# A Fourier transform ahead of two expert layers: four parity classes of the sequence index, eleven chunks instead of ten, and another order of folds

## The reference

```
X = np.fft.fft(x, axis=1)        # along the sequence, 2496 points
X = np.fft.fft(X, axis=2)        # along the features, 256 points
attn = X.real                    # (4, 2496, 256), then as 9984 rows of 256
# layer 1: logits = rows @ w_gate; every row gets one of 8 experts, at most 1248 each,
#          in the order of the largest logits; out = relu(row @ w1[e]) @ w2[e]
# layer 2: each row to its largest logit's expert, scaled by a softmax and a sigmoid gate
```

## Time and profile before

| | before |
|---|---|
| median of the runs | 1381.67 us |
| the profiled execution | 1381.85 us, of which 1380.0 us are its span |
| transform along the sequence, first to last product | 14.6 to 113.4 us |
| TensorE busy in the whole span | 93% |
| mean granted clock of TensorE | 0.929 of full speed |
| moved by the queue of SyncE in the first 60 us | 16.79 MB |

### The profile page before, as it was taken

One profiled execution on the slowest core, in us unless ns is written; L12 is line 12 of the kernel. 1 busy time (PEld: TensorE's weight loads), 2 busy tenths in 40 slices (PEclk: granted clock), 3 DMA queues, 4 the chain that ended last, 5 costly groups with the idle time before them and its releaser, 6 DMA issues.

```text
span 1380.0 us, 30713 instructions
## 1 busy us (share of the span) xinstructions
PE 1279.5 (93%) x10394; PEld 1179.9 (85%) x10395; DVE 745.8 (54%) x1994; ACT 327.8 (24%) x796; POOL 560.3 (41%) x548
## 2 busy tenths in 40 slices
PE   5999899928999998899999995999999999999996
PEld 4757788817888888789898995999999999999996
DVE  2733788896776678876445434443443433333332
ACT  0102110022322232333333321222222222222221
POOL 2800002205465656565656461421443242444411
PEclk9999755558999999999999997999999999999998
DMA  9605541003212131212222222221223122232110
GB/s 346 230 11 170 190 151 66 33 2 98 92 52 87 39 99 43 95 41 101 78 80 65 81 67 65 74 76 42 68 75 99 42 76 74 76 105 73 42 42 20
DMA packets 70729, 116.20 MB, mean 84 GB/s; under 512 B 7784, under 2 KB 50545, under 8 KB 70640
## 3 DMA queue, kind: packets, MB, share of 16 engines
q1 hardware_dynamic: 46864, 72.39, 15.7%
q0 software_dynamic: 11808, 31.03, 6.9%
q10 hardware_dynamic: 11968, 11.63, 3.0%
HBM read 81.87 MB, written 34.45 MB: 84 GB/s over the span
## 4 chain that ended last, share of the span: by engine, by line
PE 73%; DVE 11%; issue 2%; DMA 1%; ACT 1%; POOL 0%; ACTq 0%; DVEq 0%; POOLq 0%; SPq 0%
PE bank L1089 22%; PE bank L1091 21%; PE bank L1090 21%; PE bank L977 3%; PE bank L960 3%; DVE hot_r L1728 2%; PE bank L1228 1%; PE bank L1101 1%; DVE hot_q L1729 1%; DVE hot_q L1727 1%; DVE hT_low L1898 1%; DVE arena L1607 1%; DVE xT_low L1891 0%; DVE arena L1672 0%; DMA arena<-in_w2a_t 0%
## 5 line engine op out<-in xcount | busy, mean ns | idle before, releaser
L1089 PE MATMUL bank<-weights_high,hT_high 128*128 (+1 forms) x1328 | 388.4, 292 | 0.0
L1091 PE MATMUL bank<-weights_high,hT_low 128*128 (+1 forms) x1328 | 378.4, 285 | 0.0
L1090 PE MATMUL bank<-weights_low,hT_high 128*128 (+1 forms) x1328 | 377.4, 284 | 0.0
L1089 PE MATMUL bank<-xT_high,weights_high 128*128 128x256 f32 (+2 forms) x1072 | 336.4, 314 | 9.1 <-DVE xT_low L1891 4.0
L1091 PE MATMUL bank<-xT_high,weights_low 128*128 128x256 f32 (+2 forms) x1072 | 331.7, 309 | 0.0
L1090 PE MATMUL bank<-xT_low,weights_high 128*128 128x256 f32 (+2 forms) x1072 | 331.0, 309 | 0.0
L1090 PEld LDWEIGHTS bank<-weights_low,hT_high 128*128 128x128 f32 x1328 | 250.5, 189 | 0.0
L1091 PEld LDWEIGHTS bank<-weights_high,hT_low 128*128 128x128 f32 x1328 | 250.4, 189 | 0.0
L1089 PEld LDWEIGHTS bank<-weights_high,hT_high 128*128 128x128 f32 x1328 | 250.1, 188 | 0.1
L1089 PEld LDWEIGHTS bank<-xT_high,weights_high 128*128 128x128 f32 x1072 | 205.1, 191 | 24.6 <-DVE hT_low L1898 7.9
L1091 PEld LDWEIGHTS bank<-xT_high,weights_low 128*128 128x128 f32 x1072 | 204.4, 191 | 11.5
(11 more groups left out here) (256 smaller groups left out, 1438.3 us busy)
## 6 DMA issues: line engine op xcount, KB each, us to landing
arena<-middle ACTq DMA_DIRECT2D x44, 258.0 KB
spectrum<-arena SPq DMA_DIRECT2D x39, 256.0 KB, 2.2
arena<-in_w2a_t SPq DMA_DIRECT2D x8, 1024.0 KB, 5.0
raw<-in_w1a SPq DMA_DIRECT2D x8, 1024.0 KB
raw<-in_w2a SPq DMA_DIRECT2D x8, 1024.0 KB
raw<-in_w1b SPq DMA_DIRECT2D x8, 1024.0 KB
raw<-in_w2b SPq DMA_DIRECT2D x8, 1024.0 KB
arena<-in_x SPq DMA_DIRECT2D x4, 768.0 KB, 4.6
```

Of the source, the lines that this page charges most:

```text
L1089: pe.matmul(out_, a[0], b[0], start=start, stop=False)
L1090: pe.matmul(out_, a[0], b[1], start=False, stop=False)
L1091: return pe.matmul(out_, a[1], b[0], start=False, stop=stop)
```

## The change

The sequence positions are sorted by n mod 4. The even positions are split once more: positions 4j (class r = 0) and 4j + 2 (class r = 1), 3 chunks of 128 each (`EC`), and the odd positions 2j + 1 are 5 chunks (`OC`); 11 chunks in all where there were 10. A load with h = 0 holds the 6 chunks of even positions, one with h = 1 the 5 chunks of odd ones. The host lays `x`, `x_rev` and the tables out in that order, so that a partition's part of a load is one contiguous piece. (Frequencies up to an eighth of the sequence are 0 to 312, `KQ` = 313 of them; `KREST` = 312.)

A unit with h = 0 is now 3 + 3 products, 313 wide, which hold the two even classes up to frequency 312; their sum (`plus`) and difference (`minus`) are the even positions' part at k and at 624 - k. A unit with h = 1 is 5 products of the odd positions for k up to 312 and 5 for k from 313 to 624. So a pair (b, q) takes 16 products. ScalarE copies one bank for a unit with h = 0 and none for one with h = 1. VectorE does two operations behind a unit with h = 0 and four behind one with h = 1 (and the one-column one for q = 0). TensorE waits for `even` or `odd` of the load that a unit reads, no longer for both loads of a sequence. GpSimd waits for `even` of load 0 only at its load 0, where it waited for load 1's at load 0 and load 3's at load 2. The first cosine piece is loaded behind the first x load; `const` and the gate weights move from behind the fourth load to behind the sixth; `tables` moves from behind unit 7 to behind unit 12.

```
+KQ = QUARTER + 1                   # 313
+KREST = QH + 1 - KQ                # 312
+EC = QUARTER // P + 1              # 3
+OC = -(-QH // P)                   # 5
+PARTS = ((0, 2 * EC), (2 * EC, 2 * EC + OC))
+PIECE_AT = (0, 2 * EC * KQ, (2 * EC + OC) * KQ, (2 * EC + OC) * KQ + OC * KREST)
+    evens = [4 * (c * P + m) + r for r in (0, 2) for c in range(EC)]
+    return np.concatenate(evens + [2 * (c * P + m) + 1 for c in range(OC)], 1)
-        FOLDS_AT = {1: (2, 3), 3: (4,), 5: (5,), 7: (6,), 9: (7,)}
+        FOLDS_AT = {1: (2,), 2: (3,), 4: (4,), 5: (5,), 7: (6,), 8: (7,)}
+        TABLES_AT = 12
...
         @block.sync
-                sp.dma_start(xlow[:, u, 0:c1 - c0],
-                             x[b, rows].rearrange("(c p q) d -> p c q d", p=P, q=2)).then_inc(s_low[u], 16)
+                sp.dma_start(xlow[:, u, 0:c1 - c0], x[b, :, c0:c1]).then_inc(s_low[u], 16)
+                sp.dma_start(xmir[:, u, 0:c1 - c0], x_rev[b, :, c0:c1]).then_inc(s_mir[u], 16)
+                if n == 0:
+                    sp.dma_start(cosb[0], table_piece(cos_n, 0)).then_inc(s_cos[0], 16)
                 if n == 1:
-                    for h, (k0, k1) in enumerate(SPANS):
-                        for q in range(2):
-                            sp.dma_start(cosb[:, q, :, k0:k1], cos_n[:, q, :, k0:k1]).then_inc(s_cos[h], 16)
...
+                    for i in (1, 2):
+                        sp.dma_start(cosb[i], table_piece(cos_n, i)).then_inc(s_cos[i], 16)
+                    a = spot["sin"][0]
+                    sp.dma_start(sinb[0], table_piece(sin_n, 0)).then_inc(s_sin[0], 16)
+                    sp.dma_start(arena[:, a + PIECE_AT[1]:a + PIECE_AT[3]],
+                                 sin_n[:, PIECE_AT[1]:PIECE_AT[3]]).then_inc(s_sin[1], 16)
-                if n == 3:
+                if n == 5:
                     sp.dma_start(cst[:], const).then_inc(s_const, 16)
...
         @block.gpsimd
-                if n in (0, 2):
-                    pool.wait_ge(s_even, n + 2)
+                if n == 0:
+                    pool.wait_ge(s_even, 1)
...
         @block.tensor
-                if q == 0 and h == 0:
-                    pe.wait_ge(s_even, 2 * (b + 1))
-                    pe.wait_ge(s_edge, 2 * (b + 1))
-                if q == 1 and h == 0:
-                    pe.wait_ge(s_odd, 2 * (b + 1))
+                if q == 0:
+                    pe.wait_ge(s_even, 2 * b + h + 1)
+                    pe.wait_ge(s_edge, 2 * b + h + 1)
+                if q == 1:
+                    pe.wait_ge(s_odd, 2 * b + h + 1)
...
                 for r in range(2):
-                    for c in range(NC):
+                    piece, chunks_ = ((0, range(r * EC, (r + 1) * EC)), (1 + r, range(2 * EC, NC)))[h]
+                    if b == 0 and q == 0 and not (h == 0 and r):
+                        pe.wait_ge(s_cos[piece], 16)
+                    if b == 0 and q == 1 and r == 0:
+                        pe.wait_ge(s_sin[h], 16)
+                    w = KREST if piece == 2 else KQ
+                    for c in chunks_:
...
         @block.scalar
-                if n >= 3:
-                    act.wait_ge(s_seq, n - 2)
-                act.copy(half[0:m, n % 3, 0:w], bank[2 * (n % 3)][0:m, 0:w]).then_inc(s_half, 1)
+                if h == 0:
+                    if n >= 4:
+                        act.wait_ge(s_seq, n - 3)
+                    act.copy(quarter[0:m, n // 2 % 2], bank[2 * (n % 3)][0:m, 0:KQ]).then_inc(s_half, 1)
...
         @block.vector
             def joined(n):
+                if h == 0:
+                    dve.wait_ge(s_half, n // 2 + 1)
+                    dve.wait_ge(s_other_ps, n + 1)
+                    dve.tensor_tensor(add, part, two[:, 0:KQ], ALU.add)
...
+                    ins.then_inc(s_seq, 1)
+                    return
...
+                dve.wait_ge(s_half_ps, n + 1)
+                dve.tensor_tensor(to[:, 0:KQ], add, one[:, 0:KQ], ALU.add)
+                mirrored(to[:, HALF - KQ + 1:HALF - low + 1], add[:, KQ - 1:stop:-1], one[:, KQ - 1:stop:-1])
...
+                dve.wait_ge(s_other_ps, n + 1)
+                dve.tensor_tensor(to[:, KQ:QH + 1], sub[:, KREST - 1::-1], two[:, 0:KREST], ALU.add)
+                mirrored(to[:, QH + 1:QH + KREST], sub[:, 1:KREST], two[:, KREST - 2::-1]).then_inc(s_seq, 1)
-                if n == 7:
+                if n == TABLES_AT:
                     tables()
```

More of the change, by code:

```diff
@@ L204, in build_program @@
         middle = nc.dram_tensor("middle", (E * REG + W2, ROW), F32, kind="Internal").ap()
[L207 to L210, removed]
+        CP = max(b - a for a, b in PARTS)
+        sizes = [("cos", PIECE_AT[3]), ("sin", PIECE_AT[3]), ("even", NC * B * P), ("odd", NC * B * P),
+                 ("quarter", 2 * KQ), ("pad", PAD), ("seqA", B * HALF), ("seqB", B * HALF), ("xlow", 2 * CP * D), ("xmir", 2 * CP * D),
+                 ("sum", CP * D), ("dif", CP * D), ("mid_col", NC * B),
+                 ("plus", 2 * KQ), ("minus", 2 * KQ)]
         at, spot = 0, {}
@@ L222, in fft, with trig @@
             return v.rearrange(pattern, **kw) if pattern else v
[L224 to L228, removed]
-        seqA, seqB = fft("seqA"), fft("seqB")
[L230 to L234, removed]
+        def trig(name):
+            t = fft(name)
+            return [t[:, PIECE_AT[i]:PIECE_AT[i + 1]].rearrange("p (c k) -> p c k", k=KREST if i == 2 else KQ) for i in range(3)]
+        cosb, sinb = trig("cos"), trig("sin")
+        even = fft("even", "p (b c d) -> p b c d", b=B, c=NC)
+        odd = fft("odd", "p (b c d) -> p b c d", b=B, c=NC)
+        mid_col = fft("mid_col", "p (c b) -> p c b", c=NC)
+        seqA, seqB = fft("seqA"), fft("seqB")
+        xlow = fft("xlow", "p (u c d) -> p u c d", u=2, c=CP)
+        xmir = fft("xmir", "p (u c d) -> p u c d", u=2, c=CP)
+        fsum, fdif = fft("sum", "p (c d) -> p c d", c=CP), fft("dif", "p (c d) -> p c d", c=CP)
+        quarter, plus, minus = (fft(n, "p (u k) -> p u k", u=2) for n in ("quarter", "plus", "minus"))
         NST = 6
@@ L386, in build_program @@
         s_mir = [sem(f"s_mir{u}") for u in range(2)]
[L387 removed]
+        s_cos, s_sin = ([sem(f"s_{n}{h}") for h in range(w)] for n, w in (("cos", 3), ("sin", 2)))
         s_even, s_edge, s_odd = sem("s_even"), sem("s_edge"), sem("s_odd")
@@ L1499, in joined @@
                 b, q, h = work_list[n]
-                k0, k1 = SPANS[h]
-                w, m = k1 - k0, (B if q == 2 else P)
-                one, two = half[0:m, n % 3], bank[2 * (n % 3) + 1][0:m]
+                m, u = (B if q == 2 else P), n // 2 % 2
+                add, sub = plus[0:m, u], minus[0:m, u]
+                one, two = bank[2 * (n % 3)][0:m], bank[2 * (n % 3) + 1][0:m]
+                if h == 0:
+                    dve.wait_ge(s_half, n // 2 + 1)
+                    dve.wait_ge(s_other_ps, n + 1)
+                    part = quarter[0:m, u]
+                    dve.tensor_tensor(add, part, two[:, 0:KQ], ALU.add)
+                    if q == 1:
+                        ins = dve.scalar_tensor_tensor(out=sub, in0=part, scalar=-1.0, in1=two[:, 0:KQ],
+                                                       op0=ALU.mult, op1=ALU.add)
+                    else:
+                        ins = dve.tensor_tensor(sub, part, two[:, 0:KQ], ALU.subtract)
+                    ins.then_inc(s_seq, 1)
+                    return
@@ L1520, in joined @@
-                if q == 0 and h == 0:
-                    ins = dve.tensor_tensor(lastA[:, b:b + 1], one[:, 0:1], two[:, 0:1], ALU.subtract)
-                ins.then_inc(s_seq, 1)
+                dve.wait_ge(s_seq, n)
+                dve.wait_ge(s_half_ps, n + 1)
+                dve.tensor_tensor(to[:, 0:KQ], add, one[:, 0:KQ], ALU.add)
+                stop = low - 1 if low else None
+                mirrored(to[:, HALF - KQ + 1:HALF - low + 1], add[:, KQ - 1:stop:-1], one[:, KQ - 1:stop:-1])
```

84 lines of the change are left out of this document (35 added, 49 removed).

## The result

| | before | after |
|---|---|---|
| median of four runs | 1381.15 us | 1366.46 us |
| ratio, 95% interval | | 0.9892 (0.988 to 0.9905) |
| profiled execution, its span | 1381.85, 1380.0 us | 1367.67, 1365.9 us |
| first product of the stage | 14.64 us | 9.99 us |
| first feature product (the stage's end) | 113.45 us | 97.56 us |

Forecast were 1367.7 us and a stage end of 99.4. The stage gave 15.9 us, 1.9 more than the 14.0 of the forecast, and the rest of this execution was 1.8 longer than before.

A forecast was written before the change was run, and what follows sets the result against it. TensorE was taken to bound the stage. Terms -18.9 - 4.4 + 4.9 + 3.3 + 1.7, with 0.6 less for faster loading, gave -14.0: 1381.85 - 14.0 - 0.2 = 1367.7 us, 8-in-10 range 1361 to 1373.

The forecast's parts named there:

- 36 products less: TensorE in the stage: 144 products for 180 at 0.526 us each, 18.9 us less if TensorE stays the bound.
- first product earlier: Stage start: load 0's fold and the first cosine piece let TensorE start at 10.2 us, 4.4 us earlier.
- behind until unit 4 starts (loads 1 and 2): TensorE waits for load 2's even fold, ready about 34.6 us: 4.9 us lost, 0.6 less with faster loading.
- behind at unit 5 (load 3): TensorE waits for load 3's even fold, ready at 41.1 us behind GpSimd's odd fold: 3.3 us lost.
- low clock: TensorE behind the wait at unit 5: the lower clock level for part of 5 us, 1.7 us lost, taken once.
- The bound: Stage before the change: TensorE never idles once started, 0.526 us a product; VectorE and GpSimd hide.
- The turns: VectorE and GpSimd folds with all operands in SBUF run one behind the other, 13.75 us a sequence.
- 15.1 for whole lone durations: Folds of a sequence if the loser is blocked for whole instructions: 15.1 us, stage 2 to 3 us later.
- 98 to 100 named as a sign: Stage end: feature products starting from 98 to 100 us would show the forecast right.
- Behind the stage: Feature stage, turned weights and search: nothing depends on an absolute time, so no cost was counted there.
- D: Rival in the follow-up runs: the change costs 1.8 us behind the stage; no chance given.
- Joins, copies and later constants: VectorE's joins, 8 us more, hide under TensorE (0 to 2 us if not); fewer copies nothing; later constants worth 0 to 0.5.

The follow-up runs named there:

- e3_gp_waits: Changed kernel, but GpSimd waits at load 2 for VectorE's second fold of load 3, as before the change; stage end 97.7 us, program 1368.09 us.
- e2_late_cos: Changed kernel with the first cosine piece loaded behind load 1 again; first product at 12.69 us, stage end 95.8 us, program 1364.88 us.
- e1_twenty: Changed kernel with products issued once more in the even units, so a pair has 20 again; stage end 108.6 us, program 1376.38 us.
- e7_again: Changed kernel once more, unchanged, on chip 0; stage end 97.3 us, program 1360.31 us.
- e10_changed: Changed kernel unchanged, on chip 4 beside two variants; stage end 95.9 us, program 1364.71 us, ratio to before 0.9888.
- e4_short_gp: Changed kernel with GpSimd's folds cut to a few columns, half the transform left out, same products; stage end 89.3 us, program 1358.98 us.
- e8_sine_and_wait: Changed kernel with the last sine piece behind load 2 and GpSimd waiting at load 3 for VectorE's second fold; stage end 93.7, program 1359.26 us.
- e9_vector_takes_difference: Changed kernel with the last sine piece behind load 2 and VectorE making the first difference from load 2 on; stage end 91.9, program 1359.08 us.
- e5_filler: Changed kernel with six overwritten products more ahead of the sixth unit's wait for load 3's fold; stage end 95.7 us, program 1360.96 us.

## Why the prediction was right

Term by term, in us of the stage's end, from the profiled executions:

| term | forecast | in the trace |
|---|---|---|
| 36 products less | -18.9 | -18.9 |
| first product earlier | -4.4 | 9.99 - 14.64 = -4.65 |
| behind until unit 4 starts (loads 1 and 2) | +4.9, less 0.6 | 32.20 - (9.99 + 2.6 + 32 x 0.526) = +2.8 |
| behind at unit 5 (load 3) | +3.3 | 38.64 - (32.20 + 3.16) = +3.3 |
| low clock | +1.7 | 58.92 - 57.3 = +1.6 from unit 5 to the end |
| sum | -14.0 | -15.9 |

- **The bound.** Right: TensorE without a gap before, and 0.526 us a product in both kernels.
- **The turns.** Right in place and size: GpSimd's subtraction of load 2 took 5.00 us and VectorE's fold 4.06, the numbers of the earlier trace rows; e3_gp_waits shows that at units 4 and 5 the turns make the waits and not the loads. The loser was blocked as the Trainium skill has it (SBUF — State Buffer, Who interferes with whom): the fold that takes 0.95 us alone took 4.06 beside GpSimd's. The folds of loads 2 to 7 took 26.29 to 67.46 us, 41.2, which is 13.7 a sequence as forecast. The forecast's 15.1 for whole lone durations is a slip: it scales the 1.59 us of the earlier trace rows, which is not a lone duration. The lone ones of e3_gp_waits (1.76, 0.95, 1.49 and 0.82 on VectorE, 3.44, 1.80, 2.88 and 1.53 on GpSimd) add up to 14.7, so the blocking for whole instructions, as that page has it, would give 1 us a sequence too much here, not 1.4.
- **The mis-sized term** is the one for load 2. I had it land at 28.2 to 28.8 us with 375 to 395 GB/s; it landed at 26.3, since the queue moved 421 GB/s from 10 to 26 us. That is the 2 us by which the stage was earlier than forecast; it also put the first feature product, 97.6, just outside the 98 to 100 named as a sign. That the longer runs are the reason was not tested by itself.
- **How the terms add** was right in the sum and would mislead one who read it term by term: the earlier start and the wait for load 2 are two sides of one thing. e2_late_cos gives back 2.7 us of the start for nothing, and e1_twenty shows the products worth 11.0 rather than 18.9 where the waits are counted with them. From load 2 on the end is set by its landing and the turns behind it. So the -18.9 and the +2.8 of the table are a way of counting, not prices of single parts.
- **The clock.** The 1.7 us behind unit 5 came in the profiled execution and in e7_again and not in e10_changed or e2_late_cos. That it came in the profile that the forecast is held against was luck; it should have been taken in part. That a low clock behind the first wait costs nothing was right: e10_changed had it there. The Trainium skill (TensorE: Matmul & The Clock Gate, HAM oscillation) describes a kernel whose waits for data, longer than those here, each brought the low clock back; here no profile had it behind more than one of its waits.
- **Behind the stage** I counted nothing. The 1.8 us of the profiled execution are within what the same kernel varies by (1261.2 to 1268.3), but the medians speak for a cost of about 1 us or more (see D above), so this term is probably missing, and it hid part of the better stage in the total.
- Joins, copies and later constants cost nothing in the changed kernel: with e4_short_gp, which has them all, the stage ends at the sum of start and products. In e3_gp_waits and e8_sine_and_wait, with later folds, joins did hold TensorE up, by 1.5 to 2.2 us a time.

## What to carry to other kernels

Where two engines feed a third and their operations run one behind the other, as those with all operands in SBUF did here, add them up as one queue from the moment its data lands. A different order only moved the wait; an earlier landing shortened it, and giving an operation to the engine that does it in half the time ended it. A cut in the bounding engine's work brings its full price only until it meets the next queue; price the parts of a change together, by what each unit waits for last, not one by one.

## What the runs showed of the hardware

- The same first difference of 1536 columns took 3.42 us on GpSimd and 1.75 on VectorE (after, e9_vector_takes_difference); an operation of VectorE with one operand in PSUM ran at 0.47 us beside GpSimd, one with both in SBUF was held for up to 3.1 us (4.06 instead of 0.95).
- One queue moved 421 GB/s from 10 to 26 us with runs of 5 KB and more a partition (after), against 354 to 370 from 12 to 27 us with the tables in pieces of 1.25 KB (before).
- TensorE's granted clock fell to the lower of its two levels (0.50, 1.2 GHz) behind an idle of 1.88 us in e10_changed and of 3.00 us in after and e7_again, and stayed at 1.00 behind idles of 3.00 us in e2_late_cos, 2.50 in e10_changed and 2.35 in e5_filler.
- The span behind the stage, some 1265 us, differed by 7 us between three profiles of one kernel (1261.2 to 1268.3), two of them on different chips; the end of the stage differed by at most 0.3 us apart from the clock.
